# When the weights of the last layer are split into high and low parts: six blocks moved against the steps around a phase boundary

## The reference

```python
x = attention(q, k, v)                 # 2304 tokens x 512
h = x @ w_in                           # 512 -> 2048
g = s * maximum(h, 0) ** 2 + b
o = g @ w_out                          # 2048 -> 512
a, b2 = o @ w_a, o @ w_b               # 512 -> 1536 each
y = (a * b2) @ w_out2                  # 1536 -> 512
```

## Time and profile before

| | |
|---|---|
| median of 3 runs | 1062.18 us (1062.08 to 1064.16) |
| the profiled execution | 1062.08 us, its span 1060.3 us |
| PE busy | 1011.1 us, 95% of the span |
| PE weight load busy | 946.2 us, 89% |
| DVE, ACT, POOL busy | 442.5, 356.8, 159.4 us |
| mean granted PE clock | 0.982 of full |

### The profile page before, as it was taken

One profiled execution on the slowest core, in us unless ns is written; L12 is line 12 of the kernel. 1 busy time (PEld: TensorE's weight loads), 2 busy tenths in 40 slices (PEclk: granted clock), 3 DMA queues, 4 the chain that ended last, 5 costly groups with the idle time before them and its releaser, 6 DMA issues.

```text
span 1060.3 us, 17004 instructions
## 1 busy us (share of the span) xinstructions
PE 1011.1 (95%) x6984; PEld 946.2 (89%) x6984; DVE 442.5 (42%) x800; ACT 356.8 (34%) x791; POOL 159.4 (15%) x126
## 2 busy tenths in 40 slices
PE   5778899999999999999999999999999999999997
PEld 4557889999999999999999899899899998998996
DVE  4768665565565655555336441211212212112111
ACT  3535444453334533444335331211211212212211
POOL 4645443122331223220000000000000000000000
PEclk9859999999999999999999999999999999999999
DMA  8344401221021210200124330100100100100000
GB/s 195 87 116 113 126 20 50 46 69 47 13 57 46 69 46 13 57 12 24 31 87 145 112 90 1 42 19 1 61 1 1 60 1 1 60 1 1 31 1 30
DMA packets 98829, 52.50 MB, mean 50 GB/s; under 512 B 60384, under 2 KB 92768, under 8 KB 98752
## 3 DMA queue, kind: packets, MB, share of 16 engines
q1 hardware_dynamic: 98608, 51.35, 17.7%
q10 hardware_dynamic: 144, 0.07, 0.0%
HBM read 41.97 MB, written 9.44 MB: 48 GB/s over the span
## 4 chain that ended last, share of the span: by engine, by line
PE 87%; DVE 5%; ACT 3%; POOL 3%; issue 2%; DMA 1%; SPq 0%; ACTq 0%; DVEq 0%; POOLq 0%
PE bank L669 29%; PE bank L634 18%; PE bank L619 18%; PE bank L683 13%; PE bank L548 2%; PE bank L495 2%; PE bank L519 1%; PE bank L469 1%; PE bank L480 1%; DVE relu L992 1%; POOL sm L1071 1%; PE bank L540 1%; POOL sm L1079 1%; ACT sm L715 1%; PE bank L514 1%
## 5 line engine op out<-in xcount | busy, mean ns | idle before, releaser
L669 PE MATMUL bank<-x_hi,wx 128*128 128x384 f32 x1152 | 306.0, 336 | 6.5 <-DVE x_lo L986 4.0
L634 PE MATMUL bank<-g_hi,wx 128*128 128x288 f32 x1024 | 234.2, 305 | 1.4 <-DVE o_sb L1004 1.4
L619 PE MATMUL bank<-wx 128*128 128x288 f32 x1536 | 232.2, 300 | 0.4 <-ACT relu L794 0.4
L669 PEld LDWEIGHTS bank<-x_hi,wx 128*128 128x128 f32 x1152 | 209.4, 188 | 12.0 <-issue 9.1
L619 PEld LDWEIGHTS bank<-wx 128*128 128x128 f32 x1536 | 213.1, 191 | 3.4 <-issue 2.6
L669 PE MATMUL bank<-x_lo,wx 128*128 128x384 f32 x576 | 192.9, 335 | 0.0
L634 PEld LDWEIGHTS bank<-g_hi,wx 128*128 128x128 f32 x1024 | 171.8, 189 | 9.5 <-issue 4.2
L1047 DVE TENSOR_TENSOR prod<-bank,a_sb 128x384 f32<-128x384 f32 x72 | 40.2, 558 | 306.7 <-ACT a_sb L852 306.7
L634 PE MATMUL bank<-g_lo,wx 128*128 128x288 f32 x512 | 151.4, 296 | 0.0
L992 DVE SCALAR_TENSOR_TENSOR relu<-relu,s_col 128x288 f32<-128x288 f32 x128 | 81.7, 638 | 166.5 <-ACT relu L794 166.3
L852 ACT ACTIVATE a_sb<-bank 128x384 f32<-128x384 f32 x72 | 35.4, 492 | 299.9 <-PE bank L669 299.9
(11 more groups left out here) (67 smaller groups left out, 824.8 us busy)
## 6 DMA issues: line engine op xcount, KB each, us to landing
nat<-in_q SPq DMA_DIRECT2D x32, 144.0 KB, 2.9
nat<-in_k SPq DMA_DIRECT2D x32, 144.0 KB, 3.2
vnat<-in_v SPq DMA_DIRECT2D x32, 144.0 KB
o_transposed<-o_sb SPq DMA_DIRECT2D x8, 576.0 KB, 3.2
o_raw<-o_transposed SPq DMA_DIRECT2D x6, 768.0 KB, 4.6
out<-y SPq DMA_DIRECT2D x18, 256.0 KB, 2.2
vwin<-in_v SPq DMA_DIRECT2D x32, 120.0 KB
raw<-in_moe_w_a SPq DMA_DIRECT2D x12, 256.0 KB, 3.0
```

The lines of the kernel that those rows point to most:

```text
L619: mm = nc.tensor.matmul(HB[:, 0:HALF], wi(w, kd, f), xs(x, c % 2)[:, kd], start=(kd == 0 and j == 0), stop=(kd == KD - 1 and j == 2))
L634: mm = nc.tensor.matmul(ACC[o][:, 0:HALF], wo(w, f, o), g[:, slot % GB, :], start=(f == 0 and j == 0), stop=(f == F1 - 1 and j == 2))
L669: mm = nc.tensor.matmul(dst[:, 0:CH2], wab(w, f, j * KD + kd), x[:, kd, :], start=(kd == 0 and m == 0), stop=(kd == KD - 1 and m == 2))
```

## The change

Six blocks of weights are split at other places in the lists of ACT and DVE, and SP's list follows.

- Blocks 6, 7 and 8 are split right after the last slot of phase 1 and ahead of `take_acc` of the last chunk, back to back.
- Blocks 9, 10 and 11 are split in steps 0, 1 and 2 of phase 2, at the head of the step, ahead of the copy of a (ACT) and of `prod` (DVE). Before, block 6 + f stood at the end of step f.
- SP loads blocks 0 to 10, then stores the last chunk, then loads block 11.

```diff
 # SP
-            for f in range(EARLY2 + RB):          # EARLY2 = 6, RB = 3
+            for f in range(F2 - 1):               # F2 = 12
                 load_block2(f)
             store_o(NCH - 1)
-            for f in range(EARLY2 + RB, F2):
-                load_block2(f)
+            load_block2(F2 - 1)
 # ACT, after the last slot of phase 1
+            for f in range(6, 9):
+                split_w2_hi(f)
             take_acc(NCH - 1)
...
                 for f in range(F2):
                     step = F2 * c + f
+                    if c == 0 and 9 + f < F2:
+                        split_w2_hi(9 + f)
                     act.wait_ge(ab_ready, step + 1)
...
-                    if c == 0 and EARLY2 + f < F2:
-                        split_w2_hi(EARLY2 + f)
 # DVE, after the last slot of phase 1
+            for f in range(6, 9):
+                split_w2_lo(f)
             take_acc(NCH - 1)
...
                     step = F2 * c + f
+                    if c == 0 and 9 + f < F2:
+                        split_w2_lo(9 + f)
                     dve.wait_ge(a_ready, step + 1)
...
-                    if c == 0 and EARLY2 + f < F2:
-                        split_w2_lo(EARLY2 + f)
```

More of the change, by code:

```diff
@@ L48 @@
 STAGES = 3
-EARLY2 = 6
 def build(nc, q, k, v, w_in, w_out, s, b, w_a, w_b, w2, mask_in, identity, out, o_dram):
```

## The result

The changed kernel takes 1070.47 us (median of 5 runs, 1068.77 to 1073.02). The kernel before, run in between on the same chip and counted with its earlier runs, takes 1063.38 us (5 runs, 1062.08 to 1064.16). The ratio is 1.0072 with an interval of 1.0053 to 1.0090: slower by 7.7 us (5.6 to 9.6). The profiled execution took 1069.81 us, its span 1068.0 us, 7.7 us longer than the span of before.

A forecast was written before the change was run, and what follows sets the result against it. PE was taken as the bound, 87% of the chain that ended last. A 4.1 us stall plus 1.7 us of slow clock on 1062.1 us gave 1067.9 us, 0.55% slower; own range 1066.5 to 1069.3, outer 1065.4 to 1070.8.

The forecast's parts named there:

- the load of block 9: Ahead of step 0's prod: load waits for low 6, then high 9 and low 9; step 1 starts 4.1 us later.
- the rival with a longer low clock or a late block 9: At step 1: whole step at half rate, or block 9 landing late; 1070.4 or 1069.9 us, chance 0.16.
- The first branch: Step 1 runs wholly at the low clock, costing 4.2 us instead of 1.7; 1070.4 us.
- The second: Block 9 lands only 5.9 us after its third DMA: 6.1 us delay plus 1.7 for the clock, 1069.9 us.
- No split costs anything before, so nothing can be saved: Phase 2 of the kernel before: no PE wait names a weight split, so moving splits can save nothing.
- Blocks 6, 7 and 8: Phase boundary: 6 and 7 fill idle time and cost nothing; 8 lands after 5.0 us, DVE's take_acc ends at 601.8.
- Blocks 10 and 11, the store, SP: Around steps 1 and 2: block 10 hidden with 1.4 us to spare; block 11, the last store and SP cost nothing.
- The clock: PE's idle gap before step 1 drops its clock to half rate; costs 1.7 us, bounds 0 to 4.2.
- stall-alone rival: Between steps 0 and 1: PE pays 4.1 us and the clock holds; 1066.2 us, chance 0.13.
- not-slower rival: At high 9 on ACT: block 9 is there in time, so nothing on the chain differs; 1062.1 us, chance 0.05.
- The rival of a long low clock: Step 1 runs wholly at the low clock, 4.2 us instead of 1.7; 1070.4 us, chance 0.16 shared with late block 9.
- The sum: Whole kernel: 4.1 us stall plus 1.7 us clock, 5.8 us over the profiled 1062.08 us, so 1067.9 us.

The follow-up runs named there:

- e2: The changed kernel with block 9 never loaded; its split reads what block 6 left in the staging buffer and waits for no load; ratio 1.0047 to the kernel before.
- e3: The changed kernel with 26 more matmuls (the filler) between the first and second up_2, into a PSUM bank nobody reads; ratio 1.0049 to the kernel before.
- e8: The changed kernel with DVE's low parts of blocks 9 to 11 at the end of steps 0 to 2, high parts still at the head; ratio 1.0044.
- e1: The changed kernel with blocks 9, 10 and 11 split at the end of steps 0, 1 and 2, not at the head; ratio 1.0034 to the kernel before.
- e5: The changed kernel with a second pair of PSUM banks for a and b2 in phase 2, used in turn; ratio 0.9992 to the kernel before.
- e6: The changed kernel with SP's old order: blocks 0 to 8, the last chunk's store, then blocks 9 to 11; ratio 1.0113 to the kernel before.

## Why the prediction was right in its mechanism and too small in one term

The step that failed is the load of block 9. The prediction has the block there 4.9 us after its first issue (0.96 us to the third DMA and the median landing of 3.9 us), and so step 1 4.1 us late; the trace has 6.0 us and 5.3 us. The path itself (low 6, load, high 9, low 9, `prod`), the second wait at 1.3 us and the fall of the clock in the gap, and only there, are as forecast.

The measured 1070.47 us lies above the forecast's own range (1066.5 to 1069.3) and within the outer one (1065.4 to 1070.8). It also meets the number of the rival with a longer low clock or a late block 9 (1070.4), and that is chance. The first branch needed step 1 wholly at the low level, 4.2 us, and it paid 1.3. The second needed the third DMA of block 9 to land after 5.9 us, and it took 4.59.

**No split costs anything before, so nothing can be saved.** Right: from step 2 on both traces take 454.0 us.

**Blocks 6, 7 and 8.** Right for 6 and 7. Block 8 was taken from the earlier trace rows at 5.0 us; in the changed kernel's profile it took 3.8. Over the ten profiles the value goes from 3.4 to 5.3 us, and both kinds of execution have a delay: where block 8 is late, DVE's own list makes it (e2, 3.8 us; e3, 3.6 us, where the way through the load of block 9 ends level with it; forecast 3.6), where block 9 is late, its load does.

**Block 9, the term that was mis-sized.** Forecast: issued at 595.9, third DMA 0.96 us later, landing 3.9 us after it, 4.1 us of delay. Measured, from its own step 0: 5.3 us. The three issues took 1.41 us to the third (597.00 to 598.41, since the second held SP for 0.95 us and not 0.51), and the landing 4.59 us. From first issue to last landing that is 6.0 us, against 4.9 in the forecast. The forecast had another number in hand: block 8, the load nearest in time, had 6.0 us from first issue to last landing. It cited it and took the median of all twelve. With 6.0 the delay comes out at 5.2. The other profiles in which this load is issued at the same place have 4.3 (e3), 4.7 (e8), 5.3 (e1, where nothing on the path waits for it) and 5.8 us (e5). So 4.9 lies among the five values, on their lower side, and 6.0 is the highest of them: the nearest transfer would have given the delay of this one execution partly by luck. The bounds that the prediction gave for this step, 3.6 to 6.1 us of delay, hold the measured 5.3. The estimate from the Trainium skill's page "DMA: Bandwidth & Descriptors", 3.8 us, is below all five.

**Blocks 10 and 11, the store, SP.** Right: the second wait for `prod` is still 1.3 us, and from step 2 on nothing differs. That the load of block 9 goes out ahead of the store is needed for this: in e6 it stands behind it and PE waits 12.0 us.

**The clock.** Right: it fell in the gap and step 1 paid 1.31 us; forecast 1.7, the range 0 to 4.2. The other kernels with a gap paid 1.46 to 2.04 us (e5, e8, e1, e2, e6; against the 4.40 or 4.42 us of 24 matmuls behind a wait at the upper level), and 0 with the filler. This agrees with what was cited from the Trainium skill's page "TensorE: Matmul & The Clock Gate", section "Part 1: The HAM clock gate", that the slow clock is the default and activity releases it: e3 gave it activity and kept it. The prediction's argument that one gap of 1.91 us was enough is weaker than it looks; the last section has a gap of 1.91 us that lost nothing. The stall-alone rival (1066.2) and the not-slower rival are out. The rival of a long low clock is out too: the clock was back before step 1 ended.

**The sum.** Forecast 4.1 + 1.7 = 5.8 us; in the trace from step 0 on 5.3 + 1.3 = 6.6; by the ratio 7.7 (5.6 to 9.6). The rest of the difference in the two profiles, 1.06 us, lies in phase 1 and is scatter. The forecast of 1067.9 us is 2.6 us under the measured median. Some 0.8 us of it is the two terms above, and 1.3 us is the base: the sum starts from 1062.1, the profiled execution and the fastest of the five, and the kernel before had a median of 1063.38 us in these five runs. What is left, 0.5 us, is within what the intervals leave open.

Two things stay open. I do not know why the load of one block takes 4.3 us in one execution and 6.0 in the next, nor why the second issue holds SP for 0.95 to 0.97 us in some (changed, e1, e5) and for 0.51 or 0.65 in others (e3, e8). And the ratios of the timed runs differ from what the profiles from step 0 on give, by 0.8 us below (e6: 12.0 against 12.8) to 1.6 us above (e3: 5.2 against 3.6). One profile per kernel is too few to say why.

## What to carry to other kernels

Work that waits for a DMA must not be put ahead of work that the bound engine waits for, on any in-order engine, even if that engine is idle for half of the time: the two splits at the head of step 0 cost their load's wait as well. Work out the whole way of such a load from the event that frees its buffer, and carry its landing through the sum as a range, not as one median: the same load took 4.3 to 6.0 us here. And where a stall of the bound engine can't be avoided, count the clock with it, or see whether a second buffer (here two PSUM banks that lay idle) takes the waiting engine off the bound one's path.

## What the runs showed of the hardware that I had not expected

- A gap of 1.89 us on PE between dense stretches lost the clock (e1, step 1 at 6.00 us against 4.42), while the gaps of 1.26 us at the boundary did not. The fall cost 1.3 to 2.0 us each time; in e1 it cost 1.6 us where PE's wait had grown by 0.6.
- The length of the gap alone does not decide. The gap of the earlier trace rows is in e6 too, as long as before, and there the clock stayed at 1.00, where the earlier trace rows has 0.50 behind it. In e8 a gap of 1.75 us before 111.51 was followed by 0.50 from 113 to 116 us; in the kernel before, one of 1.75 us before 110.3 was not. What else decides, no run here shows.

```profile
123.47 0.71 PE L479 MATMUL bank<-pooledT 64*72 64x144 f32 x8 [1.91 <-DVE pooledT L869]
124.00:126.00 2.00, 2.00 (x18) 1.88 (x15) 1.34 (x3) 2.00 (x6) 0.00 (x0) 1.00 1.01 286
```

- The restart after a wait is not free at full clock either: 24 matmuls take 4.40 or 4.42 us after a wait and 4.18 in a stream.
- The same work of PE in phase 1 ended between 594.16 and 596.59 us in ten executions, a scatter of 2.4 us, as large as several of the effects here; all of it arose in the first 224 us.
